# Chunked linear attention with two MLPs: values asked for ahead of the rows' moves, TensorE's four-chunk tiles without a loop, weight block 2 sooner

## The reference

```python
f = 1 / (1 + exp(-f_logit))
for t in range(S):                                   # decayed linear attention
    state = f[:, :, t, :, None] * state + einsum('bhd,bhe->bhde', k[:, :, t], v[:, :, t])
    y[:, :, t] = einsum('bhd,bhde->bhe', q[:, :, t], state)
x = y as 3072 rows of 384
xn = x / sqrt(mean(x * x) + 1e-6) * rms_g            # gated MLP, 384 -> 1536 -> 384
x = (silu(xn @ w_gate) * (xn @ w_val)) @ w_out
h = x @ w_in                                         # second MLP, 384 -> 2048 -> 384
g = where(h >= 1, h, where(h <= -1, 0, (h + 1) ** 2 / 4))
out = g @ w_out2
```

## Time and profile before

| | |
|---|---|
| time before, median of 3 runs | 962.52 us (962.34 to 966.45) |
| the profiled execution's own time | 962.73 us |
| span of the profiled execution | 961.0 us |
| PE busy | 930.0 us, 97% of the span |
| DVE busy | 555.9 us, 58% |
| ACT busy | 329.2 us, 34% |
| mean granted TensorE clock | 0.995 |

### The profile page before, as it was taken

The page is one execution under the profiler, slowest core; times in us unless marked ns, Lnnn a source line. Parts: engine busy times, 40 slices in busy tenths (PEclk is TensorE's granted clock), DMA queues, the critical chain, the costliest instruction groups (busy, mean ns, idle before and its releaser), DMA issues.

```text
span 961.0 us, 18720 instructions
## 1 busy us (share of the span) xinstructions
PE 930.0 (97%) x7500; PEld 788.0 (82%) x7500; DVE 555.9 (58%) x971; ACT 329.2 (34%) x561; POOL 15.4 (2%) x35
## 2 busy tenths in 40 slices
PE   7999999799999999999999999999999999999998
PEld 4999899698877788787888878888888888888886
DVE  7987657555755574566555554545445455455443
ACT  4653223223322222222233343333333333333333
POOL 1000000000000000000000000000000000000000
PEclk9999999999999999999999999999999999999999
DMA  8622432513332233225122200000000000000000
GB/s 284 253 68 74 128 109 80 164 54 118 96 120 79 68 108 102 89 64 165 50 86 91 91 1 1 1 33 0 0 33 0 1 32 0 33 0 0 33 1 33
DMA packets 52134, 65.90 MB, mean 69 GB/s; under 512 B 14561, under 2 KB 42977, under 8 KB 52065
## 3 DMA queue, kind: packets, MB, share of 16 engines
q1 hardware_dynamic: 51920, 64.75, 21.3%
q10 hardware_dynamic: 144, 0.13, 0.0%
HBM read 51.43 MB, written 13.43 MB: 67 GB/s over the span
## 4 chain that ended last, share of the span: by engine, by line
PE 91%; issue 4%; DMA 3%; SPq 1%; DVE 1%; POOL 0%; ACT 0%; DVEq 0%; POOLq 0%; ACTq 0%
PE gate_ps L597 15%; PE val_ps L597 15%; PE acc L673 13%; PE gate_ps L661 10%; PE val_ps L661 10%; PE acc L619 9%; PE acc L677 7%; PE acc L623 4%; PE pair_ps L459 2%; PE y_ps L500 2%; PE y_ps L516 2%; DMA v_early<-v_dram 1%; DMA x_turn_dram<-x_all 1%; SPq L322 1%; PE pair_ps L505 1%
## 5 line engine op out<-in xcount | busy, mean ns | idle before, releaser
L948 ACT ACTIVATE raw<-raw,columns 128x512 f32<-128x512 f32 x96 | 69.4, 723 | 156.6 <-DVE raw L1391 156.6
L673 PE MATMUL acc<-high 128*128 128x512 f32 x282 | 109.7, 389 | 0.0
L673 PE MATMUL acc<-high,low 128*128 128x512 f32 x282 | 109.7, 389 | 0.0
L619 PE MATMUL acc<-high 128*128 128x512 f32 (+2 forms) x252 | 90.0, 361 | 0.0
L619 PE MATMUL acc<-high,low 128*128 128x512 f32 (+2 forms) x252 | 89.3, 358 | 0.0
L955 ACT ACTIVATE high<-qd 128x512 fp32r<-128x512 f32 x96 | 60.7, 632 | 73.1 <-DVE qd L1396 73.1
L677 PE MATMUL acc<-low,high 128*128 128x512 f32 x282 | 79.2, 389 | 0.0
L1391 DVE TENSOR_SCALAR raw<-val_ps 128x512 f32<-128x512 f32 x48 | 33.2, 691 | 77.5 <-PE val_ps L661 77.5
L1391 DVE TENSOR_SCALAR raw<-gate_ps 128x512 f32<-128x512 f32 x48 | 33.1, 689 | 62.7 <-PE gate_ps L661 62.7
L597 PE MATMUL gate_ps<-high 128*128 (+3 forms) x252 | 66.7, 373 | 2.4 <-DVE h_even L1309 1.5
L1328 DVE TENSOR_TENSOR low<-qd,high 128x512 fp32r<-128x512 f32 x96 | 65.7, 684 | 5.7 <-ACT high L955 5.1
(11 more groups left out here) (142 smaller groups left out, 1703.2 us busy)
## 6 DMA issues: line engine op xcount, KB each, us to landing
raw<-qkf_dram SPq DMA_DIRECT2D x22, 770.0 KB, 4.9
x_all<-wb_dram SPq DMA_DIRECT2D x12, 576.0 KB, 5.5
kd_turn_dram<-after SPq DMA_DIRECT2D x19, 256.0 KB, 3.0
kd<-kd_turn_dram SPq DMA_DIRECT2D x76, 64.0 KB, 2.4
v_sb<-v_dram SPq DMA_DIRECT2D x23, 192.0 KB, 2.5
v_early<-v_dram SPq DMA_DIRECT2D x23, 192.0 KB, 2.6
out_dram<-x_all SPq DMA_DIRECT2D x5, 768.0 KB, 3.8
x_turn_dram<-x_all SPq DMA_DIRECT2D x19, 192.0 KB, 1.9
```

The lines of the kernel that those rows point to most:

```text
L619: pe.matmul(acc[:, m, 0:width(i)], wb_part(w, j, 2, m), h_hi[:, j % 2, 0:width(i)], start=(j == 0 and w is w_hi), stop=False)
L673: pe.matmul(acc[:, m, 0:N2], wc_part(w, j, 1, m), h2_hi[:, j % 2, :], start=(j == 0 and w is w_hi), stop=False)
L948: nc.scalar.activation(act2_buf[:, j % 2, :], act2_buf[:, j % 2, :], ACT.Square, bias=half_col[:, :], scale=0.5).then_inc(square_ready, 1)
```

## The change

It has five parts:

- `tile_moves` on SP: `load_v` of the next chunk is issued behind `load_kd` and ahead of `store_x` and `load_x`, for the tile's last chunk as well.
- `gated_mlp` of tiles 3, 4 and 5 on TensorE is written out three times instead of standing in a loop. The other engines keep their loops.
- Weight block 2 is asked for behind `qd_ready` 2, ahead of the second load of `raw_second`, and no longer behind `y_made` 2. ACT splits it in tile 0's block 0, behind `sigmoid_gate(0, 0)`, and no longer before it.
- The `keep_warm(WARM_SCORES)` ahead of `attend(1, 1)` goes (`WARM_SCORES` is 1).
- `attend` is cut in two functions, with `APART` (empty) to choose where the first part stands. With `APART` empty the matmuls keep their order; the waits for `wide_ready` and `xs_ready` stand last among the waits.

```diff
+APART = {}
@@ tile_moves
                         load_raw(n + c + 1)
                         load_kd(n + c)
+                        sp.wait_ge(y_made, n + c)
+                        load_v(n + c)
                         store_x(n + c - 1)
                         load_x(n + c - 1)
-                        sp.wait_ge(y_made, n + c)
-                        load_v(n + c)
+                    if not last:
+                        sp.wait_ge(y_made, n + chunks)
+                        load_v(n + chunks)
                     store_x(n + chunks - 1)
                     load_x(n + chunks - 1)
                     if not last:
-                        sp.wait_ge(y_made, n + chunks)
-                        load_v(n + chunks)
                         sp.wait_ge(qd_ready, n + chunks + 1)
@@ SP, start
                 sp.wait_ge(qd_ready, 2)
+                load_wb(2)
                 sp.dma_start(raw_second, qkf[3]).then_inc(raw_second_loaded, 16)
                 sp.wait_ge(y_made, 2)
-                for j in range(2, 8):
+                for j in range(3, 8):
                     load_wb(j)
@@ TensorE
+                def attend_state(n, c):
+                    pe.wait_ge(wide_ready, n + 1)
+                    if n > 0:
+                        pe.wait_ge(xs_ready, n)
+                    for p in range(NP):
...
-                def attend(n, c, scores_next=False):
+                def attend(n, c, scores_next=False, state_done=False):
                     pe.wait_ge(scores_ready, n + 1)
-                    pe.wait_ge(wide_ready, n + 1)
...
+                    if not state_done:
+                        attend_state(n, c)
+                def attend_tile(i, slot, blocks):
+                    for c, due in enumerate(blocks):
+                        sooner = APART.get((i, c), 0)
+                        if sooner and slot == due - sooner:
+                            attend_state(begin(i) + c, c)
+                        if slot == due:
+                            attend(begin(i) + c, c, scores_next=c + 1 < len(blocks), state_done=sooner > 0)
@@ first_attention
                     turn_x(0, turned_x[0])
-                    keep_warm(WARM_SCORES)
                     attend(1, 1)
@@ TensorE, body
-                with pe.Fori(LOOP, TILES - 1) as i:
+                for i in range(LOOP, TILES - 1):
                     gated_mlp(i, i + 1, attention_4)
@@ ACT, gated_mlp
-                            if split and 0 < j <= JB - AHEAD:
+                            if split and j <= JB - AHEAD:
                                 split_wb(j + AHEAD - 1)
@@ ACT, body
                 round_x(0, 1, turned_x[1])
-                split_wb(2)
                 sigmoid_gate(0, 0)
```

More of the change, by code:

```diff
@@ L472, in score_alone @@
                     score(n, c)
-                def attend(n, c, scores_next=False):
+                def attend_state(n, c):
[3 more added lines that the diff above has]
+                    for p in range(NP):
+                        for s in range(C // QW):
+                            q = slice(s * QW, (s + 1) * QW)
+                            pe.matmul(y_heads[q, :, p, :], qd[0:PR, half(n, c), p, q],
+                                      wide[0:PR, p, :].rearrange("d (r e) -> d r e", r=2),
+                                      start=(p == 0), stop=False, skip_group_check=True)
+                def attend(n, c, scores_next=False, state_done=False):
                     pe.wait_ge(scores_ready, n + 1)
-                    pe.wait_ge(wide_ready, n + 1)
                     values, early = v_sb, v_early
@@ L486, in attend @@
                         pe.wait_ge(v_loaded, n * 32)
-                    if not isinstance(n, int) or n > 0:
-                        pe.wait_ge(xs_ready, n)
+                    if n > 0:
                         pe.wait_ge(state_ready, n)
-                    if not isinstance(n, int) or n >= CARRIED:
+                    if n >= CARRIED:
                         pe.wait_ge(kdT_loaded, (n - (CARRIED - 1)) * MOVED)
@@ L542, in second_tile @@
                             turn_x(n)
+                def attend_tile(i, slot, blocks):
[5 more added lines that the diff above has]
+                            attend(begin(i) + c, c, scores_next=c + 1 < len(blocks), state_done=sooner > 0)
                 def attention_3(i, slot):
-                    n = begin(i)
                     if slot == 5:
[L547 to L553, removed]
+                        score_alone(begin(i), 0)
+                    attend_tile(i, slot, BLOCKS_3)
                 def attention_4(i, slot):
-                    n = begin(i)
                     if slot == 1:
[L558 to L566, removed]
+                        score_alone(begin(i), 0)
+                    attend_tile(i, slot, BLOCKS_4)
                 def keep_warm(count):
```

## The result

The changed kernel takes 939.15 us (median of 4 runs, 938.45 to 939.61) against 963.31 us before (4 runs, 962.34 to 966.45). The ratio is 0.9743, with a 95% interval of 0.9719 to 0.9768. The forecast was 940.5 us, in a range of 937 to 947.5.

The account below looks back on a forecast made before the run. PE was taken as the bound, with 91% of the chain. From 962.7 us, less 9.4 (values), 4.4 (stall within the scores), 8.0 (jumps), 0.3 and plus 0.6 (borders), less 1.15 (start): 940.05, said as 940.5; range 937 to 947.5.

Parts of the forecast that it names:

- The values: All ten waits for the values ahead of attention blocks go: gain 9.4 us, or 1 us less where `qd` slips.
- The rival of a replaced wait: The values' wait is only replaced, by `qd` or the keys: 943.5 to 948 us; chance 0.10.
- The stall within the scores: PE's code stall at 188.2 us, in tile 2: 2.65 us goes, with 1.71 us of low clock.
- the loop's border at 11: Code border 11 instructions behind the loop's first attention block's start: no stall, so none expected at 188.2 us.
- rival A: A code border in written-out tiles 3 to 5 meets `raw` loads and stalls: 944.5 us, two 949; chance 0.20.
- The jumps: PE's two jumps back in the loop of tiles 3 to 5 go: gain 4.6 us and 3.4 of clock.
- The borders: Ends of PE's 256-instruction code blocks, moved against attention starts: two old stalls lose 0.3 us, new places cost 0.6.
- The one at 51: Tile 1, code border 51 instructions behind an attention block's start, 48 before: stall near 1.4 us, 1.55 before.
- at 67: Tile 2's first attention block, code border 67 instructions behind its start, 64 before: stall near 0.7 us, 0.89 before.
- at 45 in tile 5: Code border 45 instructions behind tile 5's second attention block's start: new stall between 0 and 1.6 us, taken as 0.6.
- The start: Tile 0: PE's second `gate` begins sooner, by weight block 2 and `keep_warm`: gain 1.15 us, bounds 0 to 1.8.
- the 0.37 us for `keep_warm`: Tile 0: without the `keep_warm` ahead of the second attention block, all moves 0.37 us forward, from 25.0 to 24.65.

Follow-up runs that it names:

- run 1: The kernel before with only the `load_v` lines of `tile_moves` moved as in the change: 947.62 us, ratio 0.9831.
- run 4: The changed kernel with TensorE's loop of tiles 3 to 5 put back: 946.38 us, ratio 0.9817.
- run 7: The changed kernel with the values of chunks 2 and later asked for between the rows' store and load: 938.94 us, ratio 0.9763.
- run 8: The changed kernel measured once more, unaltered: 939.43 us, ratio 0.9767.
- run 3: The kernel before with only weight block 2 sooner and the `keep_warm` ahead of the second attention block gone: 961.72 us, ratio 0.9974.
- run 2: The kernel before with only TensorE's loop of tiles 3 to 5 written out, the values still late: 958.56 us, ratio 0.994.
- run 6: The changed kernel with 225 more instructions (waits met at once) in PE's code of tile 0, moving the later code borders: 939.76 us, ratio 0.9766.
- run 9: The changed kernel with 31 more instructions (waits met at once) in PE's code of tile 0, moving the later code borders: 935.96 us, ratio 0.9731.
- run 10: As run 9, with `load_raw` behind `load_kd` around the first attention block of tile 2 only: 941.29 us, ratio 0.9777.
- run 5: The changed kernel with 76 more instructions (waits met at once) in PE's code of tile 0, moving the later code borders: 936.90 us, ratio 0.9736.

## Why the prediction was right

**The values: right.** 9.4 us of waits forecast and gone, in the change and alone (run 1). `qd` did not become late: in the changed kernel it is ready at 178.70, 0.6 us before the block at 179.31, close to the 0.7 us read from the earlier trace rows. The rival of a replaced wait did not come, apart from the gate's 0.65 us, which was on no list: the load of the rows landed late for ACT, and DVE's use of the gate stood behind its copy.

**The stall within the scores: right that it hangs on the values, only half right in how, and over-sized.** Of 2.65 us, 2.0 went (0.66 is left; 2.2 in run 1). I had set the rest to nothing by likeness with the loop's border at 11, but there `qd` is 3 us early and here 0.6: PE's queue had no time to run ahead. In the loop of the kernel before the fetch starts 2.6 us ahead of that block; here it starts 0.9 us behind it. Likeness of place was not enough, the queue's head start belonged to it. Nor is the queue at the wait the whole cause of the 2.65: the fetch starts behind the block in both kernels, and the part that went is the 2 us by which it started later before, with `raw`'s packets ahead of it (run 1). The prediction had `raw` only in its rival A.

**The jumps: right in time, less certain in clock.** 4.6 us gone as forecast. The clock was priced at 1.71 us for each as if it always fell. It fell behind one of two in run 1 and behind neither in the profiled execution of run 4. That all 3.4 us of it are in the difference of the two profiles is in part luck of the execution that was profiled. The whole of the loop is worth 4.8 to 7.1 us by the medians and ratios of run 4, with an interval that does not exclude the 8.0.

**The borders: right that they cost, wrong on two of three places.** The one at 51 was set at 1.4 and costs 0.9 to 1.0 in the three profiles of the changed order (result, runs 7 and 8), 1.3 and 1.6 in runs 3 and 4; at 67, 0.7 and costs 0 to 0.3; at 45 in tile 5, 0.6 and costs nothing. Run 2 has a stall of 1.44 us there when the block waits for its values. So the distance alone does not decide. What the traces show to decide is when the fetch starts: PE was on again 2.2 to 2.6 us behind the start of its packet at each of these stalls (once 3.0, in run 7). Runs 1, 2, 6 and 9 agree with that, and what delays the start (a wait of PE's queue, `raw`'s packets) is argued from the times and not separated.

**The start: 0.7 us instead of 1.15.** The step that failed is the 0.37 us for `keep_warm`. DVE bound it as forecast, free at 24.58 and PE off at 25.06. The 0.37 us did not come. POOL's `pow` did begin earlier, but it took longer and DVE went on at 20.24. DVE, POOL:

```profile
18.63 1.22 DVE L1019 TENSOR_TENSOR_SCAN after<-raw,restart_words 128x515 f32<-128x515 f32 x1
20.24 0.62 DVE L1101 SCALAR_TENSOR_TENSOR xs<-y_ps,columns,g_rows 128x384 f32<-128x384 f32 x1 [0.39 <-POOL columns L432]
...
19.15 1.05 POOL L432 TENSOR_TENSOR columns<-columns 128x1 f32<-128x1 f32 x1 [4.37 <-ACT xs L763]
```

Before, the same POOL operation took 0.67 us. In both kernels it ends 0.35 us behind DVE's scan. That it waits for the scan is my reading and was not tried.

**The sum.** From the two profiles: 19.0 us of stalls less the 2.2 that are left of them or new (0.89, 0.66 and 0.65), 5.1 of clock and 0.7 at the start make 22.6, of the 23.2 by which the span fell. Against the sum of 940.05 the profiled execution took 939.61. That it came so near is partly luck, for misses cancel: the borders cost 1.8 us less than priced and 0.6 us is unexplained, against 0.66 left of the stall in the scores, 0.65 of the gate's new wait and 0.45 missing at the start.

## What to carry to other kernels

Follow a queue of transfers for what stands idle behind someone else's round trip; a load whose buffer is free early belongs ahead of it. Then look at what a late input does beyond its own wait: here it also put the dense block behind the issue of a large load, the fetch of the next code started 2.2 us later after the block's start, and a stall two microseconds later belonged to it. And before moving a load back, list all that its reader's engine has queued behind it, for that, and not the reader, was what stopped PE in run 10.

## What the runs showed of the hardware

- Code of PE comes in blocks of 256 instructions (packets of 16,384 bytes), and within 288 dense ones the next block was late by 0.2 to 2.65 us. 76 instructions that do nothing, put in a slack place, took 2.5 us off the kernel (run 5 against run 8, same group); with 31 it was 3.5 us (run 9, another chip).
- PE was on again 2.2 to 2.6 us behind the start of the fetch's packet at those stalls (once 3.0), 2.8 us at the jumps. With `raw` (770 KB) issued 0.5 to 1.3 us ahead of the block, the packet started 4.2 to 4.5 us behind that issue (before); with the border at the same 67 instructions it started 1.4 us behind the block's start with no such load, and 3.7 with one (changed kernel). Observed, not isolated.
- A jump back in a PE loop of 1,857 instructions cost 2.26 to 2.37 us each time (before, runs 1, 3 and 4), with the values late or in time.
- The same idle time of 2.3 us in front of the same work was followed by a granted clock of 0.50 in some executions and 1.00 in others. Behind the stall in tile 2 the low clock lasted 3.41 us before, 6.83 in run 3 and 10.24 in run 2. A clock loss read from one profile is not a price for each execution.
